# Two chunks' first products alternated product by product in a three-stage attention and expert kernel

## What is computed

```python
attn = softmax(where(0 <= rel < 64, q @ k.T / 8, -1e9)) @ v      # (2, 8, 576, 64)
x = attn as (1152 tokens, 512)
p = domain_probs / sum(domain_probs)
out = sum over e of p[:, e] * (relu(x @ w1[e]) @ w2[e])          # 4 experts, 512 -> 1024 -> 512
h = out @ w_in                                                   # 512 -> 2048
result = (h * cos(h)) @ w_out                                    # 2048 -> 512, float32
```

## Time and profile before

| | us |
|---|---|
| median of 3 runs | 642.25 |
| lowest and highest | 642.09 and 642.29 |
| the profiled execution's own time | 642.59 |
| its span | 640.5 |
| TensorE matmul busy in the span | 630.0 (98%) |
| TensorE weight load busy | 562.7 (88%) |
| VectorE, ScalarE, GpSimd busy | 305.0, 259.5, 272.1 |
| granted TensorE clock | 1.0 |

### The profile page before, as it was taken

One profiled execution on the slowest core, in us unless ns is written; L12 is line 12 of the kernel. 1 busy time (PEld: TensorE's weight loads), 2 busy tenths in 40 slices (PEclk: granted clock), 3 DMA queues, 4 the chain that ended last, 5 costly groups with the idle time before them and its releaser, 6 DMA issues.

```text
span 640.5 us, 10145 instructions
## 1 busy us (share of the span) xinstructions
PE 630.0 (98%) x3656; PEld 562.7 (88%) x3656; DVE 305.0 (48%) x722; ACT 259.5 (41%) x554; POOL 272.1 (42%) x404
## 2 busy tenths in 40 slices
PE   7899999999999999999999999999999999999998
PEld 6687899999999999999999988889999999999996
DVE  6655431215433414433415433426776676756564
ACT  6685412233321233321233321246554467545542
POOL 5683336598730196730196730277000059400000
PEclk9999999999999999999999999999999999999999
DMA  9755200003220011220021220032100013001011
GB/s 290 253 178 151 104 1 1 1 23 109 67 66 1 1 65 66 65 65 0 1 65 67 67 66 1 8 117 95 46 0 1 1 33 100 1 0 49 0 51 50
DMA packets 21896, 37.25 MB, mean 58 GB/s; under 512 B 2784, under 2 KB 14048, under 8 KB 21856
## 3 DMA queue, kind: packets, MB, share of 16 engines
q1 hardware_dynamic: 20688, 36.71, 17.6%
q10 hardware_dynamic: 1168, 0.02, 0.1%
HBM read 34.36 MB, written 2.36 MB: 57 GB/s over the span
## 4 chain that ended last, share of the span: by engine, by line
PE 96%; DVE 2%; issue 1%; ACT 1%; POOL 0%; DVEq 0%
PE bank L1154 31%; PE bank L1182 31%; PE bank L1213 15%; PE bank L1199 14%; PE bank L1146 2%; PE bank L1110 1%; PE bank L1130 1%; DVE s_sb L823 1%; PE bank L1296 1%; PE bank L1338 1%; ACT prob L574 0%; DVE acc L973 0%; DVE w_hi L848 0%; DVE prob_t L838 0%; ACT x_hi L587 0%
## 5 line engine op out<-in xcount | busy, mean ns | idle before, releaser
L424 POOL TENSOR_TENSOR w_lo<-w_raw,w_hi 128x128 fp32r<-128x128 f32 (+1 forms) x252 | 150.6, 632 | 213.9 <-ACT w_hi L606 211.8
L1154 PE MATMUL bank<-x_hi,w_hi 128*128 128x384 f32 (+1 forms) x384 | 131.4, 342 | 0.2 <-DVE x_lo L852 0.2
L1154 PE MATMUL bank<-x_hi,w_lo 128*128 128x384 f32 (+1 forms) x384 | 129.1, 336 | 0.0
L1154 PE MATMUL bank<-x_lo,w_hi 128*128 128x384 f32 (+1 forms) x384 | 128.7, 335 | 0.0
L1182 PE MATMUL bank<-w_hi,hp_hi 128*128 128x512 f32 x288 | 114.8, 398 | 0.1
L1182 PE MATMUL bank<-w_hi,hp_lo 128*128 128x512 f32 x288 | 113.5, 394 | 0.0
L1182 PE MATMUL bank<-w_lo,hp_hi 128*128 128x512 f32 x288 | 112.1, 389 | 0.0
L926 DVE TENSOR_TENSOR h_raw<-bank,h_raw 128x384 f32<-128x384 f32 x84 | 46.6, 555 | 91.8 <-PE bank L1199 91.8
L1154 PEld LDWEIGHTS bank<-x_hi,w_hi 128*128 128x128 f32 x384 | 72.1, 188 | 3.6 <-issue 1.0
L1154 PEld LDWEIGHTS bank<-x_lo,w_hi 128*128 128x128 f32 x384 | 72.2, 188 | 1.6
L857 DVE SCALAR_TENSOR_TENSOR hp_lo<-bank,hp_hi 128x384 fp32r<-128x384 f32 x48 | 26.5, 555 | 98.6 <-ACT hp_hi L638 57.5
(11 more groups left out here) (103 smaller groups left out, 966.8 us busy)
## 6 DMA issues: line engine op xcount, KB each, us to landing
w_raw<-in_weights SPq DMA_DIRECT2D x43, 512.0 KB, 3.6
q_t<-in_q SPq DMA_DIRECT2D x12, 192.0 KB, 5.1
result<-acc SPq DMA_DIRECT2D x9, 256.0 KB, 2.0
w_raw<-in_weights SPq DMA_DIRECT2D x8, 256.0 KB, 5.5
k_t<-in_k SPq DMA_DIRECT2D x8, 224.0 KB, 5.7
v_w<-in_v SPq DMA_DIRECT2D x4, 384.0 KB, 4.7
v_w<-in_v SPq DMA_DIRECT2D x4, 320.0 KB, 6.4
k_t<-in_k SPq DMA_DIRECT2D x4, 192.0 KB, 3.5
```

The costliest lines, as they stand in the source:

```text
L424: last = nc.gpsimd.tensor_tensor(w_lo[:, f, at:at + part], raw[:, at - begin:at - begin + part], w_hi[:, f, at:at + part], ALU.subtract)
L1154: last = nc.tensor.matmul(ps[:, 0:TOK], w[:, f, chunk(c)], x[:, c, token_cols(t)], start=c == 0 and i == 0, stop=c == DC - 1 and i == 2)
```

## The change

Where the first products of two chunks stand together, the matmuls of the two alternate: first of A, first of B, second of A, second of B. `up_two` does this for the 40 such places; first products that stand alone, and `pe_pairs`, are as before. The waits of both chunks stand ahead of the first matmul. `up_done` is stepped by the 23rd matmul for A and by the 24th for B; before, it was the 12th and the 24th. Each matmul has the operands and the bank that it had, and their number does not change. Nothing changes on the other engines.

```diff
-            def up(f, s, n, t, after_cos):
+            def up_two(ps, f, t, ps_b, f_b, t_b):
+
+                for c in range(DC):
+                    for i, (w, x) in enumerate(((w_hi, x_hi), (w_hi, x_lo), (w_lo, x_hi))):
+                        first = nc.tensor.matmul(ps[:, 0:TOK], w[:, f, chunk(c)], x[:, c, token_cols(t)],
+                                                 start=c == 0 and i == 0, stop=c == DC - 1 and i == 2)
+                        second = nc.tensor.matmul(ps_b[:, 0:TOK], w[:, f_b, chunk(c)], x[:, c, token_cols(t_b)],
+                                                  start=c == 0 and i == 0, stop=c == DC - 1 and i == 2)
+                first.then_inc(up_done, 1)
+                second.then_inc(up_done, 1)
+
+            def ready_for_up(s, n, after_cos):
 
                 pe.wait_ge(w_lo_done, n + 1)
                 if after_cos:
                     pe.wait_ge(cos_taken, s - HB - MIX * FC + 1)
                 else:
                     pe.wait_ge(hp_lo_done, s - HB + 1)
-                up_cells(h_ps[f % HB], f, t, range(DC)).then_inc(up_done, 1)
...
             def pe_alone(e, inputs=False):
 
                 for first in range(0, FC, 2):
-                    for f in (first, first + 1):
-                        if f < 2:
-                            pe.wait_ge(pair_taken, product_count(e, GROUPS - 1, 5 + f))
-                        else:
-                            pe.wait_ge(hp_lo_done, alone(e) * FC + (f - 1))
-                        up_cells(bank[f % 2], f, NTOK - 1, range(DC)).then_inc(up_done, 1)
+                    if first == 0:
+                        pe.wait_ge(pair_taken, product_count(e, GROUPS - 1, 6))
+                    else:
+                        pe.wait_ge(hp_lo_done, alone(e) * FC + first)
+                    up_two(bank[0], first, NTOK - 1, bank[1], first + 1, NTOK - 1)
...
             def pe_turn(e, t, turn, cos=False, last=False, inputs=False):
                 for first in range(0, FC, 2):
+                    wrap = isinstance(t, int) and t == NTOK - 1
+                    next_t = 0 if wrap else t + 1
                     for f in (first, first + 1):
                         g, s = (f + LAG) % FC, turn * FC + f + LAG
                         after_cos = s - HB >= MIX * FC if isinstance(s, int) else cos
                         if f < FC - LAG:
-                            up(g, s, e * FC + g, t, after_cos)
+                            ready_for_up(s, e * FC + g, after_cos)
                         elif not last:
-                            wrap = isinstance(t, int) and t == NTOK - 1
                             if isinstance(turn, int) and MIX <= turn < MIX + NTOK - 1 and f == FC - LAG:
                                 pe.wait_ge(x2_lo_done, (turn - MIX + 2) * OC)
-                            up(g, s, (e + 1) * FC + g if wrap else e * FC + g, 0 if wrap else t + 1, after_cos)
+                            ready_for_up(s, (e + 1) * FC + g if wrap else e * FC + g, after_cos)
+                    f_a, f_b = (first + LAG) % FC, (first + LAG + 1) % FC
+                    if not last or first + 1 < FC - LAG:
+                        up_two(h_ps[f_a % HB], f_a, t if first < FC - LAG else next_t,
+                               h_ps[f_b % HB], f_b, t if first + 1 < FC - LAG else next_t)
+                    elif first < FC - LAG:
+                        up_cells(h_ps[f_a % HB], f_a, t, range(DC)).then_inc(up_done, 1)
...
                         if s == FC + LAG + 1:
                             pe.wait_ge(hp_lo_done, FC + LAG)
-                        if f < FC - LAG:
-                            up(g, s, g, t, False)
-                        elif t < NTOK - 1:
-                            up(g, s, g, t + 1, False)
+                        if f < FC - LAG or t < NTOK - 1:
+                            ready_for_up(s, g, False)
+                    f_a, f_b = (first + LAG) % FC, (first + LAG + 1) % FC
+                    if t < NTOK - 1 or first + 1 < FC - LAG:
+                        up_two(h_ps[f_a % HB], f_a, t if first < FC - LAG else t + 1,
+                               h_ps[f_b % HB], f_b, t if first + 1 < FC - LAG else t + 1)
+                    elif first < FC - LAG:
+                        up_cells(h_ps[f_a % HB], f_a, t, range(DC)).then_inc(up_done, 1)
```

## The result

| | before | changed |
|---|---|---|
| median, 15 runs each | 642.25 us | 643.67 us |
| lowest and highest | 641.78 and 643.31 | 643.01 and 644.68 |
| the profiled execution's own time | 642.59 | 643.77 |
| its span | 640.5 | 641.8 |

The ratio is 1.0019, with a 95% interval from 1.0012 to 1.0026: 1.4 us slower, and surely slower. The forecast was 643.5.

The account below looks back on a forecast made before the run. TensorE, busy 98% of the span, was taken as the bound, so only matmul distance and waits count. Terms 0 + 0.8 + 0.45 = 1.25 us took 642.25 to 643.5 us; 8-in-10 range 642.2 to 644.7.

Parts of the forecast that it names:

- Part 1: TensorE's 960 first-product matmuls in 40 blocks: alternating leaves their distance unchanged, 0 us; bounds 1.25 us either way.
- the fast rival: Alternation brings matmuls closer, first-product blocks under 4.19 us: 642.25 us, or 639.7 at 4 ns a matmul; chance 0.16.
- the rival that hung on it: The same closer-matmuls rival, at the page's isolated figure: 10.4 us gained, about 633 us; within the chance of 0.16.
- The 0.22 us step into a new bank: Second products: step into a new bank 0.22 us against a 0.229 mean; bank or moving operand left unclear.
- Part 2: A ends 1.91 us later; in expert 0's last tile this delays GpSimd's weight sums, costing 0.8 us, bounds 0 and 1.2.
- Part 3: B's waits come 2.1 us earlier; at expert 0's second tile TensorE waits for chunk 10's lo part, costing 0.45 us.
- the queue passes: TensorE's wait instructions are passed ahead of the matmuls, so they were costed at nothing.
- Part 4: Cosine layer's chain, moved by 1.91 us, still fits its 8.31 us beat with 1.2 to spare; nothing lost.
- The slack at the turn end: Cosine layer: VectorE's first `acc` operation ends about 613.8, TensorE's load comes about 0.2 before 614.55; 0.4 us left.
- The sum: Whole kernel: 0 + 0.8 + 0.45 = 1.25 us later, median from 642.25 to 643.5 us.

Follow-up runs that it names:

- order_undone: Changed kernel with the matmul order of before (all of A, then all of B), keeping the change's signals and waits: 643.67 us, ratio 1.0023.
- both_undone: Changed kernel with two of its 40 blocks, in expert 0's second and third tiles, back in the order, waits and signals of before: 642.31 us, ratio 1.0001.
- second_alternated: both_undone with the second products of all chunks but a tile's first alternating over three banks at every matmul: 642.34 us, ratio 0.9998.
- weights_first: Changed kernel with weights 1's hi part moved ahead of A's hi part in ScalarE's list, in expert 0's last tile: 642.61 us, ratio 1.0006.
- wait_last: Changed kernel with the wait for chunk 10's lo part put last of six ahead of the first block of expert 0's second tile: 643.47 us, ratio 1.0017.
- gap_after: Changed kernel with two idle VectorE writes ahead of the output additions at the cosine layer's five inner turn ends: 645.41 us, ratio 1.0047.
- gap_before: Kernel before the change with two idle VectorE writes ahead of the output additions at the cosine layer's five inner turn ends: 642.09 us, ratio 0.9997.
- gpsimd_later: Changed kernel with GpSimd's first sum of x held back until chunk 10's lo part is done: 643.85 us, ratio 1.0028.

## Why the prediction was right, and where not

- *Part 1, no change in the distance of matmuls: right.* The blocks are 4.19 us, and order_undone and both_undone put alternation at 0, from the side of the cost and from that of the gain. The step from bank to bank in the earlier trace rows had pointed this way ahead; the mean of 40 such steps in the same trace, 173.2 against 173.3 ns, would have left the fast rival little. The Trainium skill's figure for isolated matmuls ("TensorE: Matmul & The Clock Gate", section "Back-to-back issue gap"; 162.5 ns) was not reached, and the rival that hung on it is out.
- *The 0.22 us step into a new bank*, which I had put down to bank or operand and which fed the fast rival: neither, by second_alternated. What does make it is open; as a sum it costs nothing.
- *Part 2, A's end 1.91 later: right,* and the path as written: hi part of A, weights 1, GpSimd, weight sums, third pair product. GpSimd's shift was forecast at 1.61 us and its idle time is 1.60. Predicted 0.8, measured 0.88, of which 0.63 and not half falls at the second pair product; weights_first shows the path by cutting it.
- *Part 3, B's wait earlier: the mechanism right, the size low.* The term was 0.46 from a release-to-load time of 0.13; it measured 0.6, since the load came 0.33 behind. The step that failed is the sentence that cost the waits at nothing because "the queue passes" them: that held only where no wait was late. By wait_last, those that stand behind the late one are paid after it, 0.22 us for two.
- *Part 4, no loss in the cosine chain: right.* The slack at the turn end was forecast at 0.4 us, and the addition does end 0.39 ahead of the load; but the forecast left out the 0.11 from release to load, and gap_after fits the 0.28 that remain. gap_before shows that before there was more.
- *The sum:* 1.25 predicted, 1.46 by the aligned traces, 1.42 by the medians. Both terms came out low and none cancelled another, so the near hit is not luck. The Trainium skill's rule in "Perfetto Trace Analysis", section "Optimizing Tensor Performance", that a group's evacuation should overlap the next group's matmuls, had the sign right; but A's later evacuation cost in 1 block of 40, and there by the work behind it in ScalarE's list. In the others the 4.12 us of second products cover it.

## What to carry to other kernels

Where matmuls stand in an unbroken row, as here, changing the order in which they fill banks moved only the times at which banks are done and are claimed. So cost such a change by its signals and waits: go through each queue of the other engines for what stands behind the signal that comes later, above all work for a much later stage. Look again at the places that lose nothing but come close, and take the time from release to load off their slack: the next change will find them. Where several waits stand ahead of one instruction, put the one that is met last at the end.

## What the runs showed of the hardware

- TensorE's rate did not depend on how often the bank changes: 173.3 ns a matmul of 384 columns with every step in one bank or every step between two, and 4.12 us for 18 matmuls of 512 columns with three banks in turns of three or of one.
- A met wait behind a late one cost about 0.11 us on TensorE (changed kernel and gpsimd_later 0.33 us from release to load with two of them behind, wait_last 0.11 with none).
- The first six steps of a block of 384-column matmuls behind 512-column ones took 171 to 185 ns, the others 173, in both kernels; behind the first stall every step from the second on took 172 to 174. The cause is open.
- VectorE's small copy behind the lo part takes 1.59 us in the changed kernel and 0.16 when GpSimd's sum is held back (rows of gpsimd_later); GpSimd's sum ran from 85.30 to 87.16, the copy from 85.61 to 87.20. TensorE lost nothing by it here.
